# Chained comparisons in a routing kernel's rank counts, with GpSimd's low parts in pieces and seven y products a group

## The reference, cut to what matters

```python
x = attention(q, k, v)                 # 2 batches, 8 heads, 768 rows, window 128 and 4 sinks
y = ((x @ w_a) * (x @ w_b)) @ w_out    # 512 -> 1536 -> 512
logits = y @ w_gate                    # 8 experts
order = np.argsort(-logits.flatten())  # greedy: best (token, expert) pair first,
                                       # each token once, each expert at most 192 tokens
out[mask_e] = np.maximum(y[mask_e] @ w1[e], 0) @ w2[e]
```

## Time and profile before

| what | us |
|---|---|
| median of 3 runs | 654.3 (653.21 to 659.14) |
| profiled execution, its own time | 657.73 |
| its span, first to last instruction | 655.9 |
| TensorE busy | 634.5 |
| VectorE busy | 314.2 |
| ScalarE busy | 259.1 |
| GpSimd busy | 315.3 |

### The profile page before, as it was taken

How to read it: one execution, slowest core, us unless ns; L and a number is a source line. 1 busy time by engine, 2 the same in 40 slices (tenths; PEclk the granted TensorE clock), 3 DMA queues, 4 the chain that set the end, 5 groups by cost and what they waited for, 6 DMA issues and landing times.

```text
span 655.9 us, 12803 instructions
## 1 busy us (share of the span) xinstructions
PE 634.5 (97%) x4702; PEld 528.6 (81%) x4702; DVE 314.2 (48%) x1085; ACT 259.1 (40%) x633; POOL 315.3 (48%) x223
## 2 busy tenths in 40 slices
PE   8999997899999999999999999999989999999996
PEld 5666665799899989988997777777788889888894
DVE  4888665111114314751988998888811211112110
ACT  5888676233333333323232223322333432444330
POOL 7555445345545445544564653000085557765561
PEclk7999998999999999999999999999989999999999
DMA  8364210144464445435413242411659557765400
GB/s 259 108 265 144 80 58 24 51 121 128 129 194 128 123 132 170 125 105 187 128 29 118 63 137 76 146 49 49 218 208 366 201 198 271 281 251 205 178 25 24
DMA packets 76092, 94.32 MB, mean 144 GB/s; under 512 B 4448, under 2 KB 53888, under 8 KB 75392
## 3 DMA queue, kind: packets, MB, share of 16 engines
q1 hardware_dynamic: 73696, 86.82, 39.6%
q0 software_dynamic: 2048, 6.29, 3.0%
q10 hardware_dynamic: 288, 0.41, 0.2%
HBM read 87.16 MB, written 6.34 MB: 143 GB/s over the span
## 4 chain that ended last, share of the span: by engine, by line
PE 78%; POOL 10%; issue 9%; DVE 2%; DMA 1%; ACT 0%; POOLq 0%; ACTq 0%; DVEq 0%
PE bank L1208 14%; PE bank L1088 14%; PE bank L1300 13%; PE bank L1090 12%; PE bank L1089 12%; POOL pn_sb L499 7%; PE bank L1321 4%; PE bank L1100 2%; PE bank L1247 1%; PE bank L1163 1%; PE bank L1285 1%; POOL wl_ab L489 1%; DVE yhl L915 1%; DMA yg<-y_rows,idx 0%; PE bank L1176 0%
## 5 line engine op out<-in xcount | busy, mean ns | idle before, releaser
L489 POOL TENSOR_TENSOR wl_ab<-raw_ab,wh_ab 128x1024 fp32r<-128x1024 f32 x48 | 114.6, 2389 | 114.0 <-ACT wh_ab L592 114.0
L1088 PE MATMUL bank<-xh,wh_ab 128*128 128x384 f32 x384 | 133.7, 348 | 3.0 <-POOL wl_ab L489 3.0
L1090 PE MATMUL bank<-xh,wl_ab 128*128 128x384 f32 x384 | 129.5, 337 | 0.0
L1089 PE MATMUL bank<-xl,wh_ab 128*128 128x384 f32 x384 | 129.3, 337 | 0.0
L554 POOL TENSOR_TENSOR w2l<-w_raw,w2h 128x1024 fp32r<-128x1024 f32 x32 | 75.1, 2375 | 45.3 <-ACT w2h L698 45.3
L1300 PE MATMUL bank<-xgT,w_sb 128*128 128x192 f32 x512 | 88.1, 331 | 0.9 <-DVE xgT L964 0.9
L1300 PEld LDWEIGHTS bank<-xgT,w_sb 128*128 128x128 f32 x512 | 85.0, 193 | 2.0 <-issue 1.0
L839 DVE TENSOR_TENSOR hid<-hid,bank 128x384 f32<-128x384 f32 x48 | 26.6, 554 | 123.4 <-ACT hid L642 123.3
L642 ACT ACTIVATE hid<-bank 128x384 f32<-128x384 f32 x48 | 23.6, 492 | 146.4 <-PE bank L1090 146.4
L1088 PEld LDWEIGHTS bank<-xh,wh_ab 128*128 128x128 f32 x384 | 72.6, 189 | 10.6 <-issue 5.6
L499 POOL TENSOR_SCALAR pn_sb<-pe_sb,inv 128x260 f32<-128x260 f32 (+2 forms) x48 | 50.2, 1046 | 52.5 <-DVE inv L789 52.4
(11 more groups left out here) (141 smaller groups left out, 1014.7 us busy)
## 6 DMA issues: line engine op xcount, KB each, us to landing
w_sb<-in_moe_w_dram SPq DMA_DIRECT2D x8, 2048.0 KB, 7.7
w_raw<-in_moe_w_dram SPq DMA_DIRECT2D x32, 512.0 KB, 7.3
raw_ab<-in_moe_w_a_dram SPq DMA_DIRECT2D x48, 256.0 KB, 2.9
raw_ab<-in_moe_w_b_dram SPq DMA_DIRECT2D x48, 256.0 KB, 3.3
raw_out<-in_moe_w_out_dram SPq DMA_DIRECT2D x24, 256.0 KB, 2.7
lb<-logit_rows SPq DMA_DIRECT2D x4, 1536.0 KB, 6.5
v_sb<-in_v_dram SPq DMA_DIRECT2D x8, 384.0 KB
woT<-in_moe_w_outT_dram SPq DMA_DIRECT2D x1, 3072.0 KB, 11.3
```

The source lines that it names most:

```text
L489: pool.tensor_tensor(wl_ab[s % 2][:, :], raw_ab[s % 3][:, :], wh_ab[s % 2][:, :].bitcast(F32), ALU.subtract).then_inc(abl_done, 1)
L1088: pe.matmul(dst, lh, rh, start=first, stop=False)
L1089: pe.matmul(dst, lh, rl, start=False, stop=False)
L1090: return pe.matmul(dst, ll, rh, start=False, stop=last)
```

## The change

Three edits. (1) For the second and third tile of a chunk, the comparison with the earlier chunks adds the table of the tile before: it is a `scalar_tensor_tensor` with `lb` and the previous group's `ge`, both in SBUF, so that the third tile's table holds the sum of three. TensorE counts the earlier chunks' columns only for the third tile (`whole`), and VectorE takes the previous tile's sum off again in one more instruction behind L888. (2) GpSimd's `low_ab`, `low_h` and `low_out` are 4, 3 and 2 instructions of 256 columns; the last raises the semaphore. (3) Seven y products stand ahead of each of the 24 counts, 6, 5, 5 and 11 behind the stages of a round, and 15 at the end (`Y_PLACES`) instead of 12. By this 228 products are out at the rounds' start instead of 204, and `Z_ROUNDS` becomes 13.

```diff
--- before.py
+++ after.py
@@ -45,6 +45,7 @@
     NEG = -1.0e9 * 8.0
     SCALE = float(D) ** -0.5
     BIG = 2048
+    LOW_PARTS = 4
     SPARE = 4 * C - NF * (P // 4 - 2 * E) + (N - C) // 2
 
     FB = DM // P
@@ -55,9 +56,9 @@
     TILE = P // FG
     GROUPS = NT * E
 
-    Y_PLACES = 12
-    Y_FIRST, Y_PER_GROUP, Y_BETWEEN = 48, 6, 12
-    Y_AT_STAGE = [7, 6, 6, 12]
+    Y_PLACES = 15
+    Y_FIRST, Y_PER_GROUP, Y_BETWEEN = 48, 7, 12
+    Y_AT_STAGE = [6, 5, 5, 11]
     STAGES = [(256, 8), (32, 8), (4, 8), (1, 4)]
     Y_ROUNDS = Y_FIRST + Y_PER_GROUP * TC * E + Y_BETWEEN
     Z_ROUNDS = -(-Y_ROUNDS // (3 * TY))
@@ -486,8 +487,11 @@
                 pool.wait_ge(abh_done, s + 1)
                 if s >= 2:
                     pool.wait_ge(ab_ready, s - 1)
-                pool.tensor_tensor(wl_ab[s % 2][:, :], raw_ab[s % 3][:, :], wh_ab[s % 2][:, :].bitcast(F32),
-                                   ALU.subtract).then_inc(abl_done, 1)
+                for j in range(LOW_PARTS):
+                    at = slice(j * 2 * KD * P // LOW_PARTS, (j + 1) * 2 * KD * P // LOW_PARTS)
+                    low = pool.tensor_tensor(wl_ab[s % 2][:, at], raw_ab[s % 3][:, at],
+                                             wh_ab[s % 2][:, at].bitcast(F32), ALU.subtract)
+                low.then_inc(abl_done, 1)
 
             for g in range(DUOS):
                 h = 0
@@ -506,15 +510,21 @@
                 pool.wait_ge(yhh_done, z + 1)
                 if z >= 2:
                     pool.wait_ge(y_block_done, TY * (z - 1))
-                pool.tensor_tensor(yhl[z % 2][:, :], hid[:, z % NF, CY * (z // NF):CY * (z // NF + 1)],
-                                   yhh[z % 2][:, :].bitcast(F32), ALU.subtract).then_inc(yhl_done, 1)
+                for j in range(3):
+                    at, first = slice(j * CY // 3, (j + 1) * CY // 3), CY * (z // NF) + j * CY // 3
+                    low = pool.tensor_tensor(yhl[z % 2][:, at], hid[:, z % NF, first:first + CY // 3],
+                                             yhh[z % 2][:, at].bitcast(F32), ALU.subtract)
+                low.then_inc(yhl_done, 1)
 
             def low_out(z):
                 pool.wait_ge(outh_done, z + 1)
                 if z >= 2:
                     pool.wait_ge(y_block_done, TY * (z - 1))
-                pool.tensor_tensor(wl_out[z % 2][:, :], raw_out[z % 2][:, :], wh_out[z % 2][:, :].bitcast(F32),
-                                   ALU.subtract).then_inc(outl_done, 1)
+                for j in range(2):
+                    at = slice(j * DM // 2, (j + 1) * DM // 2)
+                    low = pool.tensor_tensor(wl_out[z % 2][:, at], raw_out[z % 2][:, at], wh_out[z % 2][:, at].bitcast(F32),
+                                             ALU.subtract)
+                low.then_inc(outl_done, 1)
 
             for s in range(2, STEPS):
                 low_ab(s)
@@ -814,8 +824,16 @@
                 c, own = t // TC, P * (t % TC + 1)
                 if c > 0:
                     earlier = g[:, 0:C * c].rearrange("p (c t) -> p c t", c=c)
-                    dve.tensor_scalar(earlier, lb[:, 0:c, e, :], li, 0.0, ALU.is_ge, ALU.add,
-                                      accum_out=rank_parts[:, t, e, 0:1]).then_inc(ge_ready, 1)
+                    if t % TC == 0:
+                        dve.tensor_scalar(earlier, lb[:, 0:c, e, :], li, 0.0, ALU.is_ge, ALU.add,
+                                          accum_out=rank_parts[:, t, e, 0:1]).then_inc(ge_ready, 1)
+                    else:
+
+                        dve.wait_ge(ge_ready, rows_before(m))
+                        before = ge[(m - 1) % 4][:, 0:C * c].rearrange("p (c t) -> p c t", c=c)
+                        dve.scalar_tensor_tensor(out=earlier, in0=lb[:, 0:c, e, :], scalar=li, in1=before,
+                                                 op0=ALU.is_ge, op1=ALU.add,
+                                                 accum_out=rank_parts[:, t, e, 0:1]).then_inc(ge_ready, 1)
                 dve.scalar_tensor_tensor(out=g[:, C * c:C * c + own], in0=lb[:, c, e, 0:own], scalar=li,
                                          in1=OWN[:, C - own:C], op0=ALU.is_ge, op1=ALU.mult,
                                          accum_out=rank_parts[:, t, e, 1:2]).then_inc(ge_diag, 1)
@@ -886,6 +904,10 @@
             dve.wait_ge(ge_ready, rows_before(GROUPS))
             dve.wait_ge(ge_diag, GROUPS)
             link(dve.tensor_reduce(parts[:, :, :], rank_parts[:, :, :, :], AX.X, ALU.add))
+
+            later = parts[:, :, :].rearrange("p (c t) e -> p c t e", t=TC)[:, :, 1:TC, :]
+            link(dve.tensor_tensor(later, later, rank_parts[:, :, :, 0].rearrange("p (c t) e -> p c t e", t=TC)[:, :, 0:TC - 1, :],
+                                   ALU.subtract))
             dve.wait_ge(ge_counted, GROUPS)
             link(dve.tensor_tensor(upper[:, :, :], LATE[:, 0:NT * E].rearrange("p (t e) -> p t e", t=NT),
                                    base_rn[:, :, :], ALU.add))
@@ -1095,7 +1117,8 @@
                 if t >= TC:
                     pe.wait_ge(ge_ready, rows_before(m + 1))
                 pe.wait_ge(ge_diag, m + 1)
-                for j in range(t + 1):
+                whole = 0 if t % TC == TC - 1 else t - t % TC
+                for j in range(whole, t + 1):
 
                     mm = pe.matmul(LATE[:, j * E + e:j * E + e + 1], ge[m % 4][:, j * P:(j + 1) * P],
                                    ones16[:, 0:1], start=(m == 0 and j == 0), stop=(m == GROUPS - 1 and j == t),
```

## The result

The changed kernel takes 677.2 us (median of 6 runs), the kernel before in the same comparison 658.3: a ratio of 1.030, 95% interval 1.025 to 1.035. It is 3% slower; the forecast was 669, the range 648 to 680. The profiled execution's span is 675.2 us for 655.9, 19.3 more.

The account below looks back on a forecast made before the run. Hidden steps were taken as bound by the TensorE, ScalarE, GpSimd chain, the last comparisons by VectorE and TensorE near their limits. +12.6 us hidden and +2.1 later made +14.7: 654.3 to 669.0, range 648 to 680.

Parts of the forecast that it names:

- Pieces: Hidden-layer steps: four pieces lengthen `low_ab` by 0.45 us to 2.84; +3.3 without comparisons, +0.9 with six counts, +0.8 first two.
- two steps are one low part plus the rest: Hidden-layer steps: two steps (8.44 us) are one GpSimd run of 2.39 plus 6.05; x longer costs x/2 a step.
- Two-input comparison beside the pieces: Hidden-layer steps: comparisons hold up GpSimd's pieces; +2.9 us with one earlier chunk, +3.4 with two.
- each pushes GpSimd back by 0.85: Hidden-layer steps: each two-input comparison delays GpSimd by its length less 0.155: 0.85 us at 768 columns, 0.45 at 384.
- Wait for the first `yhl`: Behind the last hidden step: TensorE waits about 1.3 us for product 3's `yhl`, its low parts pushed back by comparisons.
- L877 and L878: VectorE ahead of the last comparisons: with pieces these two wait some 0.5 us each, so groups start 1.7 us earlier.
- The last comparisons: Last stage up to `upper`: VectorE waits for pieces at two-input comparisons; `upper` at 407.8 for 403.59, +4.2 us.
- four experts at 5.75 and four at 6.3: Last comparisons: 5.75 us an expert from VectorE's waits, then 6.3 once GpSimd's lead is used up; end at 407.0.
- Rounds: Seven rounds: 28 products fewer, taken as 0.37 us a round, -2.6 in all (bounds 0 and -6.4).
- The tail's +0.5: After the rounds: fifteen products at the end instead of twelve, with eleven instead of twelve before, +0.5 us.
- that the port does not bind: Rival, chance 0.2: pieces slip between comparisons or the new comparison doesn't take the port; +2.9 us, 657.
- That TensorE's relief decides: Rival, chance 0.15: steps follow TensorE's fewer counts if GpSimd's run with waits is under 2.9 us; -8 us, 646.

Follow-up runs that it names:

- e1: The kernel before with only GpSimd's low parts cut in pieces: 661.6 us for 656.1, ratio 1.008.
- e10: The kernel before with only ScalarE's order turned: high part of the next weights ahead of the copy to `hid`; ratio 0.998.
- e7: The changed kernel with the weights' low part (`low_ab`) whole in one instruction, the other low parts still in pieces; ratio 1.015 against the kernel before.
- e5: The kernel before with only the y products changed: seven a group and fewer in the rounds; ratio 1.007.
- e2: The kernel before with GpSimd's pieces, plus a neutral second input from PSUM in second and third comparisons, all counts kept: 662.0 us, ratio 1.008.
- e3: The kernel before with GpSimd's pieces, plus a neutral second input from SBUF in second and third comparisons, all counts kept: 673.3 us, ratio 1.025.
- e4: The kernel before with only the chained two-input comparison and its saved counts, low parts whole, six y products a group; ratio 1.011.
- e6: The changed kernel with six y products a group and the earlier numbers in the rounds: 672.7 us against 658.5, ratio 1.024.
- e8: The kernel before with chained comparisons and saved counts in the second and third chunk only, low parts whole; ratio 1.003.
- e9: e8 with ScalarE's high part of the next weights ahead of its copy to `hid`; ratio 0.999 against the kernel before.

## Why the prediction was right, and where not

The direction, the main mechanism and the range held; the sum was 4.6 us short of the profile (14.7 for 19.3, of which 1.5 lie ahead of the change), made of errors of both signs.

- *Pieces:* 0.45 us a low part forecast, 0.42 measured (2.81). Steps without comparisons 4.44 forecast, 4.43 measured; with six counts 4.58 and 4.58. The rule behind it, two steps are one low part plus the rest, is confirmed by e1 and, the other way, by e10. The first two low parts cost 1.1 us for 0.8.
- *Two-input comparison beside the pieces:* 5.07 a step forecast with one earlier chunk, 4.97 measured in the seven steps (+2.2 us for +2.9); with two, 5.51 forecast, 5.39 measured in the five steps without logits (they lie between 4.57 and 6.15), and 5.58 instead of 6.12 in the one with them (+2.3 for +3.4 in the six). The step that failed is "each pushes GpSimd back by 0.85", and that both do so in every step: it is 0.71 (and 0.32 for the 0.45 at 384 columns), and with two earlier chunks both fall into the run in three of six low parts, one in two and none in one, because VectorE is itself held by the counts. With the pieces' terms, 8.3 us in the table for the 10.5 that these sum to. What I had not seen is that without the cut this term is not only absent but negative (e7): I had taken pieces as a help to the comparison and asked only what they cost, never who was allowed to be late.
- *Wait for the first `yhl`:* 1.3 forecast, 0.96 measured.
- *L877 and L878:* 1.7 us earlier forecast, 1.65 measured (0.98 + 0.98 for 1.53 + 2.08).
- *The last comparisons:* 49.0 us from the first comparison to `upper` forecast (358.8 to 407.8), 52.0 measured (370.91 to 422.92). VectorE took 46.8 us for its eight experts (370.91 to 417.69), 5.85 each and 5.70 in the middle (376.40 to 387.81 for two), so the 5.75 of the first four held to the end. The failed step is "four experts at 5.75 and four at 6.3". The 6.3 is a slip of the sum: its own terms, 4.0 and 2.6, make 6.6, and with that the stage would have been 1.2 us longer. And GpSimd had no lead to use up. It delivered 18 products' low parts every 5.69 us from the start, which is 6.64 for the 21 that TensorE needs an expert, and the deficit showed at the end as VectorE's wait of 4.33 us for TensorE, not as longer comparisons.
- *Rounds:* -2.6 forecast, -0.1 measured. Six of the seven became 0.7 us shorter in sum (54.0 for 54.8), the last 0.6 longer (10.81 for 10.17): by the new count of products the windows put two `wl_out` and then two `yhl` parts behind each other on VectorE's chain. "0.37 a round" took VectorE's chain for shorter than it is; e5 shows the same 64.8 without any port or pieces. The tail's +0.5 was 0.1, in a stretch that varies by 3.4 us between executions, so that nothing can be said of it.
- *Rivals:* that the port does not bind is refuted by e2 against e3. That TensorE's relief decides was wrong for the change, but its condition, a low part's run under 2.9 us with waits, is just what e4 and e7 meet in the hidden steps, and there the relief comes (1.8 and 2.2 us).

Taken apart, the change is: pieces +5 us (e1); the second input, only in company with the pieces in the hidden steps and in any case in the last stage; seven products +5 alone (e5), +4 in the changed kernel (e6).

The Trainium skill ("SBUF — State Buffer", section "Who interferes with whom") says, of VectorE's two-port modes, that whoever issues first gets the shared pair for the whole instruction, and that an instruction with two SBUF inputs contends with a GpSimd instruction that reads SBUF. The rows shown agree, in both directions: 2.53 us for a comparison behind a low part, and 1.06 us a piece behind comparisons (4.24 / 4).

## What to carry to other kernels

Where two engines wait for each other's whole instructions, as here, the length of an instruction is its protection: leave the one on the critical chain whole, and let the one with room wait. Before an instruction gets a second input, ask in each stage separately who is late there; the same edit (e4) was worth -2 us in one stage and +8 in the next. And work moved from a stage bound by something else into a full one costs its full time.

## What the runs showed of the hardware that I had not expected

- A GpSimd `tensor_tensor` of 256 columns takes 0.735 to 0.75 us and the next follows 0.69 behind it: 0.14 us for each cut. One that is held hides part of its start; a comparison of 1.01 us pushed it back by 0.71.
- VectorE's two-input instruction with one input in PSUM passes beside GpSimd unhindered (1410 ns, pieces 749); with a single repeated column from SBUF it is held like any other (1640 ns, pieces 1282). So a second input in SBUF is enough, however little of it there is.
- During a wait of 2.65 us of TensorE the granted clock fell to 0.50 in e8, and stayed there for 6.8 us, in which the same 8 matmuls took 1.51 us for 0.85. In e4 and e9 the same wait (2.65 and 2.64 us) left it at 1.00.
